# Opening of an attention + two-MLP kernel: pair 0's q and k loaded half from each queue, and its single-head score tiles read unstacked operands

## The chip, the cores and the metric

The kernel runs on one core of one Trainium2 chip. The metric is the device time of one execution in microseconds (us); the time before is the median of three executions. One further execution was recorded by the hardware profiler, and all rows below come from it. Engines are named as in the profile: PE (TensorE matmuls), PEld (its weight loads), DVE (VectorE), ACT (ScalarE), POOL (GpSimd), SP (SyncE); SPq and ACTq are rows in which SP and ACT issue DMAs.

## The reference

```python
q, k, v: (4, 8, 576, 64)          # batch, heads, sequence, head dim
scores = 64 ** -0.5 * q @ k.T
thresh = max(scores) - tau
scores = where(scores >= thresh, scores, -1e9)
attn = exp(scores - max(scores)); attn /= sum(attn) + 1e-9
x = (attn @ v), heads side by side -> (2304, 512)
h = x @ w_in;  x = (s * relu(h) ** 2 + b) @ w_out          # 512 -> 2048 -> 512
h = x @ w_in2; out = (max(h, 0) + alpha * min(h, 0)) @ w_out2
```

All inputs and outputs are float32.

## The kernel before

**Precision.** Every matrix product is made of three matmuls in a fast float32 form: each operand is split in a high and a low part (`q_hi`, `q_lo`, ...), and hi·hi, lo·hi and hi·lo are accumulated in PSUM.

**Attention.** The 32 heads go in 16 pairs. One pair has nine score tiles of 128 queries by 576 keys: tiles 0 to 7 alternate between the two heads (`t.i`, with `t.head = t.i % 2`), and tile 8 (`t.of_both`, `FULL = 8`) holds the last 64 queries of both. A pair is laid out over twelve steps, `LAYOUT = ["Q", 0, 1, "K", 2, 3, "L", 4, 5, 6, 7, 8]`. At step Q PE transposes the raw q of the next pair, and ACT and DVE write `q_hi` and `q_lo`; step K does it for k; at step L the last tile of the pair before is turned. A tile goes PE (`fill`), DVE maximum (`row_max`, L788), ACT exponential (L616), DVE threshold and sum (`mask`, L796), which frees the PSUM slot. Three wide PSUM slots are used in rotation, so tile 4 of pair 0 waits for the mask of tile 2, tile 5 for that of tile 3, tile 7 for that of tile 4, tile 8 for that of tile 5, and the first tile of pair 1 for that of tile 7. POOL normalises, PE turns the normalised rows (L1038) and multiplies by v (L1072).

**Stacked and unstacked scores.** One head has only 64 rows of contraction. `fill_scores` (L967, L969) does a half tile with two matmuls of 128 rows: `q_both` and `k_twice` hold hi and lo parts above each other, and `q_pad` holds `q_hi` of one head beside zeros. These stacked copies are made by DMA inside SBUF: `stack(n, par)` on SP, eleven DMAs counted by `stacked` (`STACK = 11`) and two for `q_diag_lo` counted by `diagonal`. `fill_scores_unstacked` does a half tile with three matmuls of 64 rows straight from `q_hi`, `q_lo`, `k_hi`, `k_lo` (L938, L939, L940). In pair 0 tiles 0 to 3 are unstacked (`OPENING = 4`); tile 8 always reads `q_pad` and `q_diag_lo`.

**What sets the order.** Each engine's program is written in order, and semaphores tie them. SP's program in the opening is: load q of pair 0, tau, q and k of pair 1, `stack(0, 0)`, `stack(1, 1)`, then the loads of pairs 2 and 3. ACT starts with the load of k of pair 0 and issues v of pairs 0 and 1 and q of pair 2 between its exponentials. PE runs 14 idle transposes (`run_idle`, L1077), then waits for all seven memsets of DVE (`padded`) and for q of pair 0.

**MLPs.** After the attention, two MLP layers run over five token tiles and keep PE busy to the end; the change does not touch them.

Of the kernel before, what the change touches and what calls it, by code (L numbers as in the profile page):

```python
# [26 lines left out]
F32 = mybir.dt.float32  # L27
# [5 lines left out]
P = 128  # L33
BANK = 512
DMA = 16


def attention_mlp_mlp(nc, q, k, v, tau, w_in1, w_out1, s, b, w_in2, w_out2, alpha, out):
    B, H, S, D = q.shape
# [6 lines left out]
    LAST = S - (QT - 1) * P  # L46
# [3 lines left out]
    FULL = 2 * (QT - 1)  # L50
# [12 lines left out]
    q_pairs = q.rearrange("b (n h) s d -> (b n) h s d", h=2)  # L63
    k_pairs = k.rearrange("b (n h) s d -> (b n) h s d", h=2)
    v_pairs = v.rearrange("b (n h) s d -> (b n) h s d", h=2)

    with ExitStack() as whole, ExitStack() as attention_memory:
# [14 lines left out]
        raw_q = sb("raw_q", [P, 2, QT, P], where=fetched)  # L82
        raw_k = sb("raw_k", [P, 2, QT, P], where=fetched)
# [13 lines left out]
        q_hi = sb("q_hi", [P, 2, S], F32R, att)  # L97
        q_lo = sb("q_lo", [P, 2, S], F32R, att)
# [5 lines left out]
        q_pad = sb("q_pad", [P, 2, 2 * S], F32R, att)  # L104

        q_diag_lo = sb("q_diag_lo", [P, 2, P], F32R, att)
# [40 lines left out]
        q_in = [sem(f"q_in{i}") for i in range(2)]  # L147
        k_in = [sem(f"k_in{i}") for i in range(2)]
        v_in = [sem(f"v_in{i}") for i in range(2)]
        diagonal = [sem(f"diagonal{i}") for i in range(2)]  # L150
# [43 lines left out]
        def wait_alone(eng, sm, value):  # L194

            if not (isinstance(value, int) and value <= 0):
                eng.wait_ge(sm, value)
                eng.sem_inc(tick, 1)
# [60 lines left out]
        def static(x):  # L259
            return isinstance(x, int)  # L260
# [112 lines left out]
        block = whole.enter_context(nc.Block())  # L373


        def load(eng, raw, par, pairs, n, order, landed):

            for h in range(2):
                eng.dma_start(raw[:, par, 0:QT - 1, D * h:D * h + D],
                             pairs[bass.ds(n, 1), h, 0:S - LAST, :].rearrange(order, p=P)  # L380
                             ).then_inc(landed, DMA)

        def load_tails(eng, raw, par, pairs, n, landed):
            eng.dma_start(raw[0:LAST, par, QT - 1, :].rearrange("p (h d) -> p h d", h=2),
                         pairs[bass.ds(n, 1), :, S - LAST:S, :].rearrange("o h p d -> p (o h) d")
                         ).then_inc(landed, DMA)

        def load_raw_q(eng, n, par):
            load(eng, raw_q, par, q_pairs, n, "o (t p) d -> p (o t) d", q_in[par])
            load_tails(eng, raw_q, par, q_pairs, n, q_in[par])  # L390

        def load_raw_k(eng, n, par):
            load(eng, raw_k, par, k_pairs, n, "o (p t) d -> p (o t) d", k_in[par])
            load_tails(eng, raw_k, par, k_pairs, n, k_in[par])
# [13 lines left out]
        @block.sync  # L408
        def _(sp):
            def load_qk(n, par):  # L410
                if not (static(n) and n < 2):
                    wait_alone(sp, filled, k_filled(n - 2))
                load_raw_q(sp, n, par)
                load_raw_k(sp, n, par)

            def q_filled(n):

                return 1 if static(n) and n == 0 else Use(n - 1, Q_POS).uses + 1

            def k_filled(n):  # L420

                return 2 if static(n) and n == 0 else Use(n - 1, K_POS).uses + 1

            def stack(n, par):

                def put(dst, src, landed=stacked):
                    sp.dma_start(dst.bitcast(F32), src.bitcast(F32)).then_inc(landed[par], DMA)

                a, b, most, rest = slice(0, D), slice(D, P), slice(0, S - LAST), slice(S - LAST, S)
                wait_alone(sp, qk_hi_ok, 2 * n + 1)  # L430
                put(q_both[a, par, 0, :], q_hi[a, par, most])
                put(q_both[b, par, 1, :], q_hi[b, par, most])
                if static(n) and n == 0:
                    sp.wait_ge(padded, PADDED)
                    sp.wait_ge(diag_padded, 1)
                put(q_pad[a, par, 0:S], q_hi[a, par, :])
                put(q_pad[b, par, S:S + LAST], q_hi[b, par, rest])
                put(q_pad[b, par, S + LAST:2 * S], q_hi[b, par, most])
                wait_alone(sp, freed, q_filled(n))
                put(q_both[b, par, 0, :], q_lo[a, par, most])  # L440
                put(q_both[a, par, 1, :], q_lo[b, par, most])
                wait_alone(sp, qk_hi_ok, 2 * n + 2)
                for rows in (a, b):
                    put(k_twice[rows, par, 0, :], k_hi[a, par, LAST:S + LAST])
                    put(k_twice[rows, par, 1, :], k_hi[b, par, 0:S])
                put(q_diag_lo[a, par, 0:D], q_lo[a, par, rest], diagonal)
                put(q_diag_lo[b, par, D:P], q_lo[b, par, rest], diagonal)

            def load_v(n, par):
                wait_alone(sp, pv_done, 2 * (n - 1))  # L450
                load_raw_v(sp, n, par)

            def load_w_in1(n):
                sp.dma_start(win_raw[:, :, bass.ts(n, P)], in_chunk(w_in1, n)).then_inc(win_in, DMA)

            def in_chunk(w, n):
                return w[:, bass.ts(n, P)].rearrange("(c p) f -> p c f", p=P)

            load_raw_q(sp, 0, 0)
            sp.dma_start(tau_c[:], tau.partition_broadcast(P)).then_inc(tau_in, DMA)  # L460
            load_raw_q(sp, 1, 1)
            load_raw_k(sp, 1, 1)
            stack(0, 0)
            stack(1, 1)
            sp.wait_ge(filled, k_filled(0))
            load_raw_k(sp, 2, 0)
            load_qk(3, 1)
            with sp.Fori(1, PAIRS // 2 - 1) as it:
                for par in range(2):
                    n = it * 2 + par  # L470
                    stack(n, par)
                    load_qk(n + 2, par)
                    load_w_in1(n)
                    load_v(n, par)
            for n in range(PAIRS - 2, PAIRS):
                stack(n, n % 2)
                load_w_in1(n)
                load_v(n, n % 2)
                load_w_in1(n - (PAIRS - 2))
            sp.dma_start(s_c[:], s.partition_broadcast(P)).then_inc(const_in, DMA)  # L480
            sp.dma_start(b_c[:], b.partition_broadcast(P)).then_inc(const_in, DMA)
            sp.dma_start(alpha_rows[:], alpha.rearrange("(j p) -> j p", p=P)).then_inc(const_in, DMA)
            sp.wait_ge(filled, k_filled(PAIRS - 1))
            for number, m in enumerate(STAGED):
                kind, j = WEIGHTS[m]
                slot = number % 4
                if number >= 4:
                    sp.wait_ge(w_ok, STAGED[number - 4] + 1)
                dst = stage[:, slot, :]
                if kind == "in2":  # L490
                    sp.dma_start(dst.rearrange("p (c f) -> p c f", c=DC), in_chunk(w_in2, j)).then_inc(stage_in[slot], DMA)
                else:
                    src = w_out1 if kind == "out1" else w_out2
                    sp.dma_start(dst, src[j * P:(j + 1) * P, :]).then_inc(stage_in[slot], DMA)

            def store(i):
                for sub in range(subs(i)):
                    wait_alone(sp, y_ok[sub], i + 2)
                    sp.dma_start(out[bass.ds(i * TOK + sub * P, P), :], y_sb[:, sub, :]).then_inc(y_out[sub], DMA)

            with sp.Fori(0, FULL_TILES) as i:
                store(i)
            store(FULL_TILES)
            for sub in range(SUB):
                sp.wait_ge(y_out[sub], DMA * (1 + FULL_TILES + (sub < REST_SUB)))
# [67 lines left out]
        def _(act):  # L573
# [107 lines left out]
                    load_raw_v(act, 1, 1, [V1_AT.index(l)])  # L681

            V0_AT, Q2_AT, V1_AT = [0, 1, 2], 3, [5, 6, 7]
            load_raw_k(act, 0, 0)
            act.wait_ge(ident_ok, 2)
            nc.scalar.activation(one_exp[:], ident[:, 0:1], ACT.Exp)
            steps(act, emit)
# [247 lines left out]
        def _(pe):  # L935
# [34 lines left out]
                                              start=False, stop=True)  # L970
                mm.then_inc(filled, 1)

            OPENING, QUIET = 4, 4

            def fill_scores_unstacked(t):
                lhs = [x[t.part, t.parity, t.q0:t.q0 + P] for x in (q_hi, q_lo)]
# [101 lines left out]

            pe.wait_ge(ident_ok, 2)
            run_idle(14)  # L1080
            pe.wait_ge(padded, PADDED)

            def emit(n0, l):
                for back in (l % POS, l % POS + POS):
                    t = Use(n0, l - back)
                    if t.inside:
                        for group, c in PV.get(back, ()):
                            times_v(t.pair, t.parity, group, c)
                fill(Use(n0, l + 2), n0, l + 2)
                if static(n0) and n0 == 0 and l < QUIET:  # L1090
                    run_idle(3)
                for t in turns_at(n0, l):
                    turn(t)
# [111 lines left out]
```

## Time and profile before

| | us |
|---|---|
| median of 3 runs | 1107.29 (1106.79 to 1107.41) |
| profiled execution, its own time | 1107.03 |
| span of the profiled execution | 1105.1 |
| PE busy | 1090.8 (99% of the span) |
| DVE busy | 525.6 |
| mean granted TensorE clock | 0.998 of full speed |

The span runs from the first instruction to the last. The profile gives the busy time of each engine, a chain of waits followed back from the last instruction, and, for a stretch, the instructions of each engine in order of time, with the idle time before each and what ended it. Starts are in us from the span's start.

### The profile page before, as it was taken

The numbers are of one execution on the slowest core, as the hardware profiler recorded it, in microseconds if no ns is written. First come the engines' busy times: TensorE is split into PE (matmuls) and PEld (weight loads), VectorE is DVE, ScalarE is ACT, GpSimd is POOL, SyncE is SP. The second block draws the span as 40 slices with busy tenths as digits, with TensorE's granted clock in tenths as the row PEclk, the third lists the DMA queues.
The fourth block names the chain that finished last, engine by engine and source line by source line (L and its number), as shares of the span: only waits on it lengthen the run. The fifth ranks groups of instructions, "written<-read, shape, count | busy, mean of one in ns | idle before, by whom it ended". The sixth has DMA issues, their size and how long they took to land.

```text
span 1105.1 us, 18966 instructions
## 1 busy us (share of the span) xinstructions
PE 1090.8 (99%) x5826; PEld 892.2 (81%) x5826; DVE 525.6 (48%) x1016; ACT 507.9 (46%) x946; POOL 258.0 (23%) x438
## 2 busy tenths in 40 slices
PE   8999999999999999999999999999999999999998
PEld 7777877777688888888888889888888888888897
DVE  7888889888643332242242246522322332332232
ACT  4777878777654332232232235544433333333343
POOL 3566656566564300000000004322000000000000
PEclk9999999999999999999999999999999999999999
DMA  8666566664121100000000003311100100010010
GB/s 188 153 157 154 141 150 149 153 146 123 31 58 48 48 1 1 1 0 0 0 0 0 0 10 96 86 48 29 39 0 0 38 0 0 0 38 0 0 39 20
DMA packets 86554, 59.28 MB, mean 54 GB/s; under 512 B 49376, under 2 KB 69872, under 8 KB 86512
## 3 DMA queue, kind: packets, MB, share of 16 engines
q1 hardware_dynamic: 83248, 57.58, 20.5%
q10 hardware_dynamic: 3264, 1.18, 0.5%
q8 instruction: 22, 0.36, 0.1%
q14 instruction: 20, 0.16, 0.1%
HBM read 30.94 MB, written 4.72 MB: 32 GB/s over the span
## 4 chain that ended last, share of the span: by engine, by line
PE 93%; DVE 2%; ACT 2%; issue 1%; DMA 0%; POOL 0%; SPq 0%; ACTq 0%; POOLq 0%; DVEq 0%
PE psum L938 23%; PE psum L940 23%; PE psum L939 23%; PE psum L1072 6%; PE psum L1038 5%; PE psum L967 3%; PE psum L969 3%; PE psum L951 2%; PE psum L1067 2%; DVE act_r L874 2%; PE psum L1046 1%; ACT win_hi L593 1%; PE psum L1035 1%; ACT act_r L706 0%; DMA k_twice<-k_hi 0%
## 5 line engine op out<-in xcount | busy, mean ns | idle before, releaser
L940 PE MATMUL psum<-x_hi,win_lo 128*128 128x512 f32 (+1 forms) x640 | 238.7, 373 | 0.0
L939 PE MATMUL psum<-x_lo,win_hi 128*128 128x512 f32 (+1 forms) x640 | 238.2, 372 | 0.0
L938 PE MATMUL psum<-x_hi,win_hi 128*128 128x512 f32 (+1 forms) x640 | 238.1, 372 | 0.0
L939 PEld LDWEIGHTS psum<-x_lo,win_hi 128*128 128x128 f32 x640 | 120.2, 188 | 24.0
L938 PEld LDWEIGHTS psum<-x_hi,win_hi 128*128 128x128 f32 x640 | 120.3, 188 | 23.0
L940 PEld LDWEIGHTS psum<-x_hi,win_lo 128*128 128x128 f32 x640 | 120.2, 188 | 22.9
L885 DVE SCALAR_TENSOR_TENSOR act_r<-act_n,nalpha,act_r 128x512 f32<-128x512 f32 (+1 forms) x80 | 56.2, 702 | 160.1 <-ACT act_r L717 159.8
L874 DVE SCALAR_TENSOR_TENSOR act_r<-act_r,s_c 128x512 f32<-128x512 f32 (+1 forms) x80 | 72.4, 905 | 116.4 <-ACT act_r L706 116.4
L616 ACT ACTIVATE ex<-psum,negm 128x576 f32<-128x576 f32 x144 | 107.5, 747 | 37.9 <-DVE negm L788 36.7
L709 ACT ACTIVATE g_hi<-act_r,b_c 128x512 fp32r<-128x512 f32 (+1 forms) x80 | 54.6, 682 | 152.5 <-PE psum L940 122.4
L550 POOL TENSOR_SCALAR ex<-ex,none_in,rinv 128x576 f32<-128x576 f32 x142 | 117.5, 828 | 19.9 <-DVE rinv L807 13.0
L796 DVE SCALAR_TENSOR_TENSOR ex<-psum,thr,ex 128x576 f32<-128x576 f32 x144 | 117.1, 813 | 8.8 <-ACT ex L616 3.7
L788 DVE TENSOR_REDUCE negm<-psum 128x1 f32<-128x576 f32 x144 | 107.8, 748 | 25.7 <-PE psum L969 24.1
L877 DVE SCALAR_TENSOR_TENSOR g_lo<-act_r,b_c,g_hi 128x512 fp32r<-128x512 f32 (+1 forms) x80 | 56.4, 704 | 133.6 <-ACT g_hi L709 133.6
L938 PE MATMUL psum<-g_hi,wout_hi 128*128 128x512 f32 (+1 forms) x320 | 118.1, 369 | 1.0 <-DVE g_lo L877 1.0
L940 PE MATMUL psum<-g_hi,wout_lo 128*128 128x512 f32 (+1 forms) x320 | 118.1, 369 | 0.0
L939 PE MATMUL psum<-g_lo,wout_hi 128*128 128x512 f32 (+1 forms) x320 | 117.7, 368 | 0.0
L940 PE MATMUL psum<-wout_hi,g_lo 128*128 128x512 f32 x288 | 112.6, 391 | 0.0
L938 PE MATMUL psum<-wout_hi,g_hi 128*128 128x512 f32 x288 | 112.4, 390 | 0.0
L939 PE MATMUL psum<-wout_lo,g_hi 128*128 128x512 f32 x288 | 112.2, 390 | 0.0
L888 DVE TENSOR_TENSOR g_lo<-act_r,g_hi 128x512 fp32r<-128x512 f32 (+1 forms) x80 | 51.1, 639 | 105.8 <-ACT g_hi L720 105.8
L716 ACT ACTIVATE act_n<-psum 128x512 f32<-128x512 f32 (+1 forms) x80 | 44.3, 554 | 120.7 <-PE psum L940 120.7
(93 smaller groups left out, 1614.7 us busy)
## 6 DMA issues: line engine op xcount, KB each, us to landing
k_twice<-k_hi SPq DMA_DIRECT2D x64, 144.0 KB, 2.5
stage<-in_moe_w_out_dram SPq DMA_DIRECT2D x32, 256.0 KB, 2.6
out_dram<-stage SPq DMA_DIRECT2D x18, 256.0 KB, 2.2
q_both<-q_hi SPq DMA_DIRECT2D x32, 128.0 KB, 2.3
q_both<-q_lo SPq DMA_DIRECT2D x32, 128.0 KB, 2.3
win_raw<-in_moe_w_in_dram SPq DMA_DIRECT2D x16, 256.0 KB, 2.9
stage<-in_moe_w_in_dram SPq DMA_DIRECT2D x16, 256.0 KB, 2.6
raw_q<-in_q_dram SPq DMA_DIRECT2D x30, 128.0 KB, 2.4
```

The costliest lines, as they stand in the source:

```text
L550: nc.gpsimd.tensor_scalar(t.ex, t.ex, none_in[r, c], rinv[r, c], ALU.add, ALU.mult).then_inc(normed, 1)
L616: nc.scalar.activation(t.ex.rearrange("p (a c) -> p a c", a=2), t.wide[r, :, 0:HALF], ACT.Exp, bias=negm[r, t.col]).then_inc(exped, 1)
L788: nc.vector.tensor_reduce(negm[r, t.col], t.wide[r, :, 0:HALF], AX.XY, ALU.max, negate=True).then_inc(maxed, 1)
L796: nc.vector.scalar_tensor_tensor(out=e, in0=t.wide[r, :, 0:HALF], scalar=thr[r, t.col], in1=e, op0=ALU.is_ge, op1=ALU.mult, accum_out=rsum ...
L874: nc.vector.scalar_tensor_tensor(out=r, in0=r, scalar=s_c[:], in1=r, op0=ALU.mult, op1=ALU.mult).then_inc(t_ok, 1)
L877: nc.vector.scalar_tensor_tensor(out=g_lo[:, j % 2, 0:n], in0=r, scalar=b_c[:], in1=g_hi[:, j % 2, 0:n].bitcast(F32), op0=ALU.add, op1=ALU ...
L885: nc.vector.scalar_tensor_tensor(out=r, in0=act_n[:, j % 2, 0:n], scalar=nalpha[:, j:j + 1], in1=r, op0=ALU.mult, op1=ALU.add).then_inc(t_ ...
L938: nc.tensor.matmul(dst, lhs[0], rhs[0], start=first, stop=False)
L939: nc.tensor.matmul(dst, lhs[0], rhs[1], start=False, stop=False)
L940: return nc.tensor.matmul(dst, lhs[1], rhs[0], start=False, stop=final)
L1038: mm = nc.tensor.transpose(t.buf[:, c, :], ex[:, t.keys0 + c * P:t.keys0 + (c + 1) * P], ident[:])
L1072: nc.tensor.matmul(o_bank[part, o_cols], raw_v[:, par, h, c, :], pt[:, h, c, cols], start=(c == 0), stop=False)
```

## The change

1. **Loads of pair 0.** SP loads head 0 of q, q's tails and head 0 of k; ACT loads head 1 of q, head 1 of k and k's tails. Before, SP had all of q and ACT all of k.
2. **Scores of pair 0.** `OPENING = FULL`, so tiles 0 to 7 are all unstacked.
3. **Stack of pair 0.** Nothing reads `q_both` and `k_twice` of pair 0 any more. `short_stack` issues four DMAs of 64 columns for tile 8, two into `q_pad` and two into `q_diag_lo`, and adds the missing nine increments to `stacked` itself.
4. **PE's first wait.** PE waits for two memsets before the first transposes, and for all seven only before tile 0.

```diff
+        def load_first(eng, head, of_q=True):
+            if of_q:
+                load(eng, raw_q, 0, q_pairs, 0, "o (t p) d -> p (o t) d", q_in[0], [head])
+            else:
+                load(eng, raw_k, 0, k_pairs, 0, "o (p t) d -> p (o t) d", k_in[0], [head])
...
+            def short_stack():
+                rest = slice(S - LAST, S)
+                sp.wait_ge(padded, PADDED)
+                sp.wait_ge(diag_padded, 1)
+                for part, col in ((slice(0, D), S - LAST), (slice(D, P), S)):
+                    sp.dma_start(q_pad[part, 0, col:col + LAST].bitcast(F32),
+                                 q_hi[part, 0, rest].bitcast(F32)).then_inc(stacked[0], DMA)
+                sp.sem_inc(stacked[0], (STACK - 2) * DMA)
+                sp.wait_ge(freed, q_filled(0))
+                for h in range(2):
+                    part = slice(D * h, D * h + D)
+                    sp.dma_start(q_diag_lo[part, 0, part].bitcast(F32),
+                                 q_lo[part, 0, rest].bitcast(F32)).then_inc(diagonal[0], DMA)
...
                 wait_alone(sp, qk_hi_ok, 2 * n + 1)
+                if static(n) and n == 0:
+                    short_stack()
+                    return
                 put(q_both[a, par, 0, :], q_hi[a, par, most])
                 put(q_both[b, par, 1, :], q_hi[b, par, most])
-                if static(n) and n == 0:
-                    sp.wait_ge(padded, PADDED)
-                    sp.wait_ge(diag_padded, 1)
...
-            load_raw_q(sp, 0, 0)
+            load_first(sp, 0)
+            load_tails(sp, raw_q, 0, q_pairs, 0, q_in[0])
+            load_first(sp, 0, False)
...
-            load_raw_k(act, 0, 0)
+            load_first(act, 1)
+            load_first(act, 1, False)
+            load_tails(act, raw_k, 0, k_pairs, 0, k_in[0])
...
-            OPENING, QUIET = 4, 4
+            OPENING, QUIET = FULL, 4
...
             run_idle(14)
-            pe.wait_ge(padded, PADDED)
+            pe.wait_ge(padded, 2)
 
             def emit(n0, l):
+                if static(n0) and n0 == 0 and l == 0:
+                    pe.wait_ge(padded, PADDED)
```

On SP, between the loads of pair 1 and the loads of pair 2, the program before has both full stacks (a put is L427; the semaphores waited for stand in brackets):

```order
L427 DMA q_both<-q_hi 64x512 [waits qk_hi_ok]
L427 DMA q_both<-q_hi 64x512
L427 DMA q_pad<-q_hi 64x576 [waits diag_padded,padded]
L427 DMA q_pad<-q_hi 64x64
L427 DMA q_pad<-q_hi 64x512
L427 DMA q_both<-q_lo 64x512 [waits freed]
L427 DMA q_both<-q_lo 64x512
L427 DMA k_twice<-k_hi 64x576 [waits qk_hi_ok]
L427 DMA k_twice<-k_hi 64x576 x3
L427 DMA q_diag_lo<-q_lo 64x64 x2
L427 DMA q_both<-q_hi 64x512 [waits qk_hi_ok]
```

and the changed program has, in the same place:

```order
L437 DMA q_pad<-q_hi 64x64 [waits qk_hi_ok,diag_padded,padded]
L437 DMA q_pad<-q_hi 64x64
L443 DMA q_diag_lo<-q_lo 64x64 [waits freed]
L443 DMA q_diag_lo<-q_lo 64x64
L449 DMA q_both<-q_hi 64x512 [waits qk_hi_ok]
```

The last row of each is the first put of pair 1: it moves from behind thirteen DMAs to behind four.

On PE, the program before has tiles 4 and 5 of pair 0 as four matmuls each, the first of them behind `stacked0`:

```order
L967 MATMUL psum<-k_twice,q_both 128x288 [waits stacked0,freed]
L969 MATMUL psum<-k_lo,q_pad 128x288
L967 MATMUL psum<-k_twice,q_both 128x288
L969 MATMUL psum<-k_lo,q_pad 128x288
L967 MATMUL psum<-k_twice,q_both 128x288 [waits freed]
```

and the changed program has tile 4 and the first matmul of tile 5 as:

```order
L964 MATMUL psum<-k_hi,q_hi 128x288 [waits freed]
L965 MATMUL psum<-k_lo,q_hi 128x288
L966 MATMUL psum<-k_hi,q_lo 128x288
L964 MATMUL psum<-k_hi,q_hi 128x288
L965 MATMUL psum<-k_lo,q_hi 128x288
L966 MATMUL psum<-k_hi,q_lo 128x288
L964 MATMUL psum<-k_hi,q_hi 128x288 [waits freed]
```

Each of tiles 4 to 7 has two matmuls more, and the wait on `stacked0` has moved to tile 8.

## Rows read from the trace of the kernel before

**Rows 1.** The page: span, busy tenths of PE, granted clock, in 40 slices.

```profile
span 1105.1 us, 18966 instructions
...
PE   8999999999999999999999999999999999999998
...
PEclk9999999999999999999999999999999999999999
```

**Rows 2.** Stretches: start:end, length; busy PE, PEld, DVE, ACT, POOL; clock; DMA.

```profile
2.00:4.00 2.00, 2.00 (x12) 2.00 (x11) 1.70 (x2) 0.48 (x1) 0.00 (x0) 1.00 0.95 215
...
14.10:17.50 3.40, 2.59 (x17) 1.85 (x16) 3.15 (x8) 1.14 (x3) 1.32 (x3) 1.00 1.04 252
17.50:20.90 3.40, 3.04 (x12) 2.92 (x12) 2.73 (x8) 1.25 (x2) 1.55 (x4) 0.51 1.12 224
20.90:24.30 3.40, 2.52 (x18) 2.02 (x17) 3.40 (x9) 2.33 (x4) 2.34 (x5) 0.99 1.11 240
24.30:27.70 3.40, 2.37 (x20) 1.96 (x19) 2.88 (x10) 3.19 (x6) 2.51 (x7) 1.00 0.69 153
...
28.00:30.00 2.00, 2.00 (x18) 1.81 (x17) 1.79 (x5) 1.50 (x4) 0.98 (x4) 1.00 0.69 153
```

**Rows 3.** The chain of waits in the opening: start, us, what.

```profile
22.76 4.51 DMA k_twice<-k_hi
...
27.41 0.37 PE psum L967
```

**Rows 4.** Timeline of SP's DMA issues: start, us, engine, what, count.

```profile
11.58 2.46 SPq L427 DMA_DIRECT2D k_twice<-k_hi  x4
...
15.62 1.17 SPq L427 DMA_DIRECT2D q_both<-q_hi  x2
```

**Rows 5.** Timeline of the head: PE's weight loads and ACT's last load of k.

```profile
1.54 2.85 PEld L1077 LDWEIGHTS psum<-ident 128*128 128x128 f32 x14 [1.54 <-POOL ident L512]
...
2.72 0.77 ACTq L384 DMA_DIRECT2D raw_k<-in_k_dram  x1
...
4.84 0.93 PEld L951 LDWEIGHTS psum<-ident,raw_q 128*128 128x128 f32 x5 [0.46 <-issue]
...
6.40 1.14 PEld L951 LDWEIGHTS psum<-ident,raw_k 128*128 128x128 f32 x6
```

**Rows 6.** Timeline of ACT writing the high parts of pair 1.

```profile
9.11 0.65 ACT L627 ACTIVATE q_hi<-psum 128x576 fp32r<-128x576 f32 x1 [0.50 <-PE psum L951]
...
13.57 0.69 ACT L627 ACTIVATE k_hi<-psum 128x640 fp32r<-128x640 f32 x1
```

**Rows 7.** Timeline of DVE's maxima (L788) and masks (L796) from tile 3 on.

```profile
18.05 0.82 DVE L796 SCALAR_TENSOR_TENSOR ex<-psum,thr,ex 128x576 f32<-128x576 f32 x1 [0.24 <-ACT ex L616]
...
19.23 0.76 DVE L788 TENSOR_REDUCE negm<-psum 128x1 f32<-128x576 f32 x1 [0.35 <-PE psum L969]
...
20.30 0.76 DVE L788 TENSOR_REDUCE negm<-psum 128x1 f32<-128x576 f32 x1
20.97 0.81 DVE L796 SCALAR_TENSOR_TENSOR ex<-psum,thr,ex 128x576 f32<-128x576 f32 x1
...
25.34 0.81 DVE L796 SCALAR_TENSOR_TENSOR ex<-psum,thr,ex 128x576 f32<-128x576 f32 x1
...
28.21 0.76 DVE L788 TENSOR_REDUCE negm<-psum 128x1 f32<-128x576 f32 x1 [1.00 <-PE psum L969]
```

**Rows 8.** Timeline of PE: two matmuls of tile 3, then tiles 4 and 5.

```profile
15.53 0.29 PE L940 MATMUL psum<-k_hi,q_lo 64*128 64x288 f32 x1
15.66 0.29 PE L938 MATMUL psum<-k_hi,q_hi 64*128 64x288 f32 x1
...
17.86 0.61 PE L967 MATMUL psum<-k_twice,q_both 128*128 128x288 f32 x1 [1.17 <-DVE ex L796]
...
18.74 0.45 PE L969 MATMUL psum<-k_lo,q_pad 128*128 128x288 f32 x1
...
18.98 0.55 PE L967 MATMUL psum<-k_twice,q_both 128*128 128x288 f32 x1
```

More of the change, by code:

```diff
@@ L373, in attention_mlp_mlp, with load @@
         block = whole.enter_context(nc.Block())
-        def load(eng, raw, par, pairs, n, order, landed):
-            for h in range(2):
+        def load(eng, raw, par, pairs, n, order, landed, heads=range(2)):
+            for h in heads:
                 eng.dma_start(raw[:, par, 0:QT - 1, D * h:D * h + D],
```

## The prediction

> **What bounds the kernel now.** I read the page first: PE is eight or nine tenths busy in every slice of the 40 and its clock is full [rows 1]. So the kernel is bound by PE, and a change to the opening is worth the time by which PE's unbroken stretch starts earlier. The view by stretches shows where that begins: from 28 us on PE works 2.00 of 2.00, while from 24.3 to 27.7 it works 2.37 of 3.40 [rows 2]. The chain of waits names what holds it last: the last `k_twice` put of pair 1 takes 4.51 us from 22.76 to its landing, and the first tile of pair 1 starts behind it at 27.41 [rows 3]. The put is late because SP issues thirteen puts for pair 0 first; pair 1's first goes out at 15.62 [rows 4]. DVE is the other engine to watch: it sits idle 1.00 us before that tile's maximum at 28.21, but from 20.9 to 24.3 it works 3.40 of 3.40 [rows 2, 7].
>
> One more thing stands in the stretches, TensorE's clock: 0.51 of full from 17.5 to 20.9, so the level of 1.2 GHz, and 2.4 GHz on both sides [rows 2]. Tiles 4 and 5 and most of tile 6 fall in it. There the matmuls of a tile follow each other by 0.24 us (18.74 to 18.98), at the full level by 0.13 us (15.53 to 15.66) [rows 8].
>
> **The change part by part.** The sum is made against the profiled execution: 1107.03 us, which is the span of 1105.1 and 1.9 around it, and 0.26 below the median of 1107.29.
>
> *Head (loads of pair 0, PE's first wait).* The weight loads of PE's idle transposes end at 1.54 + 2.85 = 4.39, and q's first weights load at 4.84, 0.46 us of idleness later [rows 5]. Two waits can end there, the memsets of DVE and the landing of q's tails. Both get shorter: PE needs two memsets only, and q's tails become SP's second issue instead of its third. So q starts up to 0.45 us earlier. For k nothing improves: its tails remain ACT's third issue, at 2.72, and k's weights load at 6.40 with no idleness before them, which says only that k had landed by then [rows 5]. Bounds: nothing, if k's landing takes over at once (or a loss as small, if the interleaved loads delay k), and 0.45 if all passes through. I take 0.25, near the middle, as neither row speaks for an end.
>
> The DMA engines are already 0.95 busy from 2 to 4 us [rows 2]. The Trainium skill has a rule that speaks against this part ("DMA: Bandwidth & Descriptors", "Issuing engines are not separate DMA queues"): transfers started from several engines share the same DMA engines and save only the time of issuing. The busy share agrees. By the rule alone the split is worth nothing more than q's tails issued earlier; with no gain in the head at all the forecast would be 1106.9 instead of 1106.6.
>
> *Stack of pair 0.* Thirteen puts become four. The first put of pair 1 needs `q_hi` of pair 1, done at 9.11 + 0.65 = 9.8 [rows 6]; four puts at 0.6 each (2.46 for four [rows 4]) are out before that. So it goes out 5.8 us earlier. Pair 1's `k_twice` puts need `k_hi`, done at 13.57 + 0.69 = 14.3 [rows 6], so they are out by 14.3 + 2.46 = 16.8 and landed, even at the 4.51 of [rows 3], by 21.3. PE asks for them past 26. The wait goes with 5 us to spare, and SP's later loads move up too. What is late next: PE's own transposes before the tile, over at 27.41 - 1.03 = 26.4 (3.40 - 2.37 = 1.03 idle [rows 2]), and DVE's mask of tile 7, which frees the slot at 25.34 + 0.81 = 26.15 [rows 7]. Gain on both engines: 1.0 us.
>
> *Tiles 4 to 7 unstacked.* Eight matmuls more. Tile 4 starts at 17.86, released by DVE's mask of tile 2 and not by the stack [rows 8], so it starts no earlier but for the head. At half clock its six matmuls occupy PE until 17.86 + 0.40 + 5 x 0.24 = 19.46 (0.40 for the first, as now: 18.98 - 17.86 less 3 x 0.24), where tile 5 now starts at 18.98. Tile 5's last matmul starts at 19.46 + 5 x 0.24 = 20.66 and ends 0.45 later, at 21.1, so DVE's maximum of tile 5 moves from 20.30 to 21.14, by 0.84 [rows 7]. From there DVE works without a stop to the last mask of pair 0, so all of it shifts by 0.84, the mask of tile 7 too. Tiles 6 and 7 run at full clock again; their extra matmuls, 2 x 0.13 each, lie beside DVE's 0.76 + 0.81 per tile. With tiles 4 and 5 at full clock the price would be nothing for the same reason. That is the lower bound; the upper one is below under B. I take 0.84, since nothing in the change removes the idle time ahead of the half-clock stretch.
>
> *Sum:* -0.25 - 1.0 + 0.84 = -0.4 us, so 1107.03 - 0.4 = 1106.6.
>
> **Rivals.**
> A. *No half clock in pair 0.* For it: PE has more matmuls to do from 18 on, and the gap before 17.86 may shrink. Against it: that gap, 1.17 us, hangs on DVE's masks [rows 8]. Price: the maximum of tile 4 starts when DVE has finished mask 3, at 18.05 + 0.82 = 18.87 instead of 19.23; the maximum of tile 5 follows it at once, and the mask of tile 4 comes at 20.3 instead of 20.97 [rows 7]. DVE is unbroken from there, so 0.67 earlier. Sum: -0.25 - 1.0 - 0.67 = -1.9, so 1105.1.
>
> B. *More half clock, and slower than before.* The clock fell at 17.5, behind a stretch in which PE did tiles 2 and 3 as 64-row matmuls and then stood idle; it did not fall behind 20.9 to 24.3 or 24.3 to 27.7, where PE worked no more (2.52 and 2.37 against 2.59) but with 128-row matmuls [rows 2, 8]. The change puts 64-row matmuls in tiles 4 to 7. So the level of 1.2 GHz may last for another stretch, or come back. From 20.9 to 24.3 DVE, with 3.40 of 3.40, hides most of it: the time is about that of before. It decides when it covers the transposes and tiles from 24.3 on, where PE is what others wait for: 3.4 us at half speed lose 1.7. Sum: -0.4 + 1.7 = +1.3, so 1108.3; twice that, 1110. The Trainium skill ("TensorE: Matmul & The Clock Gate", "What's actually happening") says that the low level is the default and that activity lifts it; it says nothing there on 64 rows. By that sentence alone the added matmuls would speak for A; the three stretches just compared speak for B.
>
> C. *The wait doesn't turn into time.* The tile starts earlier, but the turning of pair 0 is then held by POOL, which normalises tiles 7 and 8 behind the threshold of pair 1's first tile. For it: DVE feeds POOL and is nearly full. Against it: that threshold moves up with the tile. The same time results if the new load order delays k, or if `short_stack` sits in SP's queue longer than reckoned. Sum: +0.0 to -0.25, so 1106.8 to 1107.3.
>
> **How the numbers follow.** The forecast 0.48 (its own range 1106.1 to 1107.2), A 0.17, B 0.20, C 0.15. What a measurement of this kernel can tell from no change is about 0.2%, 2.2 us, so "within" is 1105.1 to 1109.5. Only A with the full head gain of 0.45 passes the lower bound; with something for gains that I don't see, faster by over 0.2% has 0.12. Only B with two stretches passes the upper: 0.05. Within has 0.83. The range goes from A less a tenth, 1105.0, to B and a little more, 1108.6.
>
> **What would show it.** In the profile after: q's first weights at 4.4 to 4.6, k's at 6.1 to 6.4; SP's first put of pair 1 near 9.8 and its last `k_twice` out by 17; no wait of PE on `k_twice`; tile 4 as six matmuls from about 17.6 on, 0.24 us apart, and DVE's maximum of tile 5 near 20.9; one half-clock stretch of about 3.4 us, and the first tile of pair 1 near 27.0 instead of 27.41. That tile near 25.5, and no half clock, means A; near 28 or later, with a second half-clock stretch, B. The forecast is wrong outright if the first maximum of pair 1 moves by over 2 us either way, or if PE's rows after 28 us show waits that they don't have now.

## The result and the profile after

The changed kernel has a median of 1109.21 us (1107.51 to 1109.9, 17 runs) against 1106.9 (1106.55 to 1108.7, 17 runs) for the kernel before: a ratio of 1.0018, 95% interval 1.0011 to 1.0024. By that ratio it is slower by 2.0 us (1.2 to 2.7); the medians lie 2.3 apart. The forecast was 1106.6 in a range that ended at 1108.6, so both its sign and its range were wrong. The profiled execution took 1108.34 us, 1.3 more than that of before, so most executions lost more than the one whose rows follow.

The stretches of the changed kernel, in the columns of [rows 2], show where it went:

```profile
16.00:18.00 2.00, 1.05 (x6) 0.81 (x6) 1.68 (x6) 0.74 (x1) 1.55 (x3) 1.00 1.12 210
18.00:20.00 2.00, 1.97 (x11) 1.98 (x12) 1.10 (x4) 0.74 (x1) 0.67 (x3) 0.50 1.12 217
20.00:22.00 2.00, 1.07 (x5) 0.72 (x4) 2.00 (x5) 0.74 (x1) 1.70 (x3) 0.50 1.16 231
22.00:24.00 2.00, 2.00 (x11) 1.72 (x9) 1.51 (x6) 0.74 (x1) 0.27 (x1) 0.50 1.32 211
24.00:26.00 2.00, 2.00 (x11) 1.98 (x10) 1.15 (x6) 1.23 (x2) 1.30 (x3) 0.50 0.51 107
26.00:28.00 2.00, 2.00 (x11) 2.00 (x10) 1.90 (x5) 1.23 (x2) 1.22 (x3) 0.50 0.35 79
28.00:30.00 2.00, 2.00 (x17) 1.79 (x16) 1.30 (x4) 1.53 (x4) 0.89 (x2) 0.94 0.01 4
```

The last number but two is the clock. It is 0.50 from 18 to 28 us, ten microseconds where the profile of before had 3.4. From 22 to 28 PE is busy without a gap, at half speed. DVE works 1.51 and 1.15 of 2.00 from 22 to 26, where it was full in the kernel before:

```profile
22.00:24.00 2.00, 1.80 (x13) 1.56 (x14) 2.00 (x6) 1.29 (x3) 1.29 (x3) 1.00 1.10 226
24.00:26.00 2.00, 2.00 (x18) 1.79 (x17) 2.00 (x5) 1.79 (x3) 1.41 (x4) 1.00 0.76 163
```

PE's timeline has the transposes and the first tile of pair 0, then tile 7, the end of tile 8 and the first tile of pair 1:

```profile
1.54 3.10 PE L1103 MATMUL psum<-ident 128*128 128x128 f32 x14 [1.54 <-POOL ident L536]
4.48 0.71 PE L977 MATMUL psum<-ident,raw_q 128*128 128x128 f32 x5
...
5.94 0.84 PE L977 MATMUL psum<-ident,raw_k 128*128 128x128 f32 x6 [0.42 <-DMA raw_k<-in_k_dram]
...
8.62 0.36 PE L964 MATMUL psum<-k_hi,q_hi 64*128 64x288 f32 x1 [0.31 <-DVE k_lo L840]
...
21.41 0.60 PE L964 MATMUL psum<-k_hi,q_hi 64*128 64x288 f32 x1 [0.93 <-DVE ex L822]
...
25.26 0.44 PE L966 MATMUL psum<-k_hi,q_diag_lo 128*128 128x288 f32 x1
25.50 1.05 PE L1064 MATMUL psum<-ident,ex 128*128 128x128 f32 x4
26.35 1.27 PE L977 MATMUL psum<-ident,raw_q 128*128 128x128 f32 x5
27.41 1.45 PE L1064 MATMUL psum<-ident,ex 128*128 128x128 f32 x8
28.62 0.38 PE L993 MATMUL psum<-k_twice,q_both 128*128 128x288 f32 x1
```

The first tile of pair 1 no longer waits for any DMA, yet it starts at 28.62 instead of 27.41 [rows 3]. DVE's maxima of tiles 5, 7 and 8 and of pair 1's first tile now wait for PE, where only the last did so before [rows 7]:

```profile
19.87 0.76 DVE L814 TENSOR_REDUCE negm<-psum 128x1 f32<-128x576 f32 x1 [0.86 <-PE psum L966]
...
23.25 0.76 DVE L814 TENSOR_REDUCE negm<-psum 128x1 f32<-128x576 f32 x1 [0.49 <-PE psum L966]
...
25.74 0.76 DVE L814 TENSOR_REDUCE negm<-psum 128x1 f32<-128x576 f32 x1 [0.85 <-PE psum L966]
...
29.45 0.76 DVE L814 TENSOR_REDUCE negm<-psum 128x1 f32<-128x576 f32 x1 [0.70 <-PE psum L995]
```

SP does what was forecast: pair 1's first put goes out at 9.92 instead of 15.62 [rows 4], its `k_twice` puts are out by 17.6.

```profile
9.92 1.16 SPq L449 DMA_DIRECT2D q_both<-q_hi  x2
...
14.61 2.94 SPq L449 DMA_DIRECT2D k_twice<-k_hi  x4
```

### The profile page after: what moved, and what is told of

Its sections match the earlier page's. It is cut to its first block, busy times and chain, and to the rows that moved or that the text cites. A ratio compares the mean times of both kernels' runs of the same rounds, so it can differ in the third digit from the quotient of the medians.

```text
span 1106.5 us, 18973 instructions
## 1 busy us (share of the span) xinstructions
PE 1092.6 (99%) x5834; PEld 894.3 (81%) x5834; DVE 526.1 (48%) x1016; ACT 507.7 (46%) x946; POOL 258.0 (23%) x438
## 4 chain that ended last, share of the span: by engine, by line
PE 93%; DVE 3%; ACT 2%; issue 1%; POOL 0%; DMA 0%; ACTq 0%; POOLq 0%; DVEq 0%
PE psum L964 23%; PE psum L966 23%; PE psum L965 23%; PE psum L1098 6%; PE psum L1064 5%; PE psum L993 3%; PE psum L995 3%; PE psum L977 2%; PE psum L1093 2%; DVE act_r L900 2%; PE psum L1072 1%; ACT win_hi L617 1%; PE psum L1061 1%; ACT act_r L732 0%; DMA raw_k<-in_k_dram 0%
```

## The experiments

For every run the mean granted clock over the whole span is known. A microsecond at half clock takes half a microsecond off it, so over 1107 us a mean of 0.995 is about 11 us at half clock (10 to 12, by the rounding), 0.998 about 4, and 1.0 about 1 or less; in the traces up to 1.4 us of it lie at the very end of the kernel (e4). The changed kernel had 0.995 or 0.996 in all 17 runs. The 33 runs of the kernel before that went with e1 to e4 had 0.996 or 0.997 in 13 and 0.998 or 1.0 in 20. The 13 took no longer than the others: the medians by clock lie between 1106.8 and 1107.0. So the kernel before, too, has more than 3.4 us of half clock in some runs, and there it costs nothing.

**The unstacked tiles alone (e1).** The kernel before with:

```diff
-            OPENING, QUIET = 4, 4
+            OPENING, QUIET = FULL, 4
```

> The kernel before with OPENING = FULL alone: pair 0's tiles 4 to 7 as six 64-row matmuls, all else (loads, eleven-DMA stack) as before. Theory 64-ROW: these tiles keep TensorE's clock at half level for about 10 us, as in the profile of the changed kernel; the wait on k_twice stays but is covered, so about 1109 to 1110 us (+2 to +3). Theory LOADS (the new load order disturbs the opening): same clock as before, one half-clock stretch of 3.4 us, about 1107.0 to 1107.8.

Measured: 1108.61 against 1106.95, ratio 1.0016 (1.0007 to 1.0025), mean clock 0.995 to 0.997. Its stretches show the same half clock as those of the changed kernel:

```profile
20.00:22.00 2.00, 1.07 (x6) 0.72 (x4) 1.83 (x4) 0.74 (x1) 1.69 (x3) 0.50 0.93 286
22.00:24.00 2.00, 2.00 (x9) 1.72 (x9) 1.51 (x4) 0.74 (x1) 0.46 (x2) 0.50 0.97 226
24.00:26.00 2.00, 2.00 (x10) 1.98 (x9) 1.19 (x5) 1.23 (x2) 1.08 (x3) 0.50 0.65 143
26.00:28.00 2.00, 2.00 (x11) 2.00 (x11) 1.93 (x4) 1.11 (x2) 1.23 (x3) 0.50 0.51 119
```

This one constant brings most of the loss, somewhat less than the 2 to 3 us expected.

**The loads alone (e2).** The kernel before with the diff's `load_first`, the new order of loads and PE's shorter first wait.

> The kernel before with the new load order and PE's shorter first wait alone. Theory 64-ROW: the first tile of pair 0 starts 0.3 to 1.0 us earlier, but the first tile of pair 1 still waits for k_twice, whose puts are bound by SP's queue; 1106.4 to 1107.0 (0 to -0.5), one half-clock stretch. Theory LOADS: slower than before by over 1 us, or the long half-clock stretch appears here too.

Measured: 1107.12, ratio 1.0005 (0.9995 to 1.0014). Seven runs lie at 1106.7 to 1107.3 with a clock of 0.997 to 1.0, four at 1108.0 to 1108.4 with 0.995. So neither text is right: the loads cost nothing clear of noise, but the half clock did get longer in some runs, and the four with the lowest clock are 1 us slower. In the profiled one, at 1107.04, it lasted 6.8 us, from 19.1 to 25.9, though tiles 4 to 8 have only 128-row matmuls here:

```profile
20.00:22.00 2.00, 1.00 (x5) 0.73 (x4) 1.93 (x5) 1.15 (x3) 1.51 (x5) 0.50 1.13 273
22.00:24.00 2.00, 2.00 (x11) 1.98 (x11) 2.00 (x5) 1.17 (x3) 1.12 (x3) 0.50 1.08 223
```

PE had stood idle for 2.06 us before tile 4 and for 1.00 before tile 7. So 64 rows are not the only thing that can go with a longer half clock. The profile also shows why starting pair 0 earlier gains nothing while its stack is whole: tile 4 is ready sooner and then waits 2.06 us for its own `k_twice`.

```profile
17.99 0.37 PE L978 MATMUL psum<-k_twice,q_both 128*128 128x288 f32 x1 [2.06 <-DMA k_twice<-k_hi]
```

**Rows or count (e3, e4).** Two kernels that change only tiles 4 to 7 of pair 0. e3 keeps four matmuls per tile and gives them 64 rows; it leaves out the product hi·lo of these tiles:

```diff
+                    if static(t.pair) and t.pair == 0 and not t.of_both:
+                        nc.tensor.matmul(dst, q_hi[t.part, t.parity, cols], k_hi[t.part, t.parity, k0:k0 + HALF],
+                                         start=True, stop=False)
+                        mm = nc.tensor.matmul(dst, q_hi[t.part, t.parity, cols], k_lo[t.part, t.parity, k0:k0 + HALF],
+                                              start=False, stop=True)
+                    elif t.of_both:
-                    if t.of_both:
```

> The kernel before, with pair 0's tiles 4 to 7 as two 64-row matmuls per half (hi.hi and lo.hi, read unstacked; the product hi.lo is left out) in place of two 128-row ones: as many matmuls of as many columns as before, at the same places and behind the same waits, only with 64 rows. Theory 64-ROW: the half-clock stretch grows from 3.4 us to 7 or 10 us, 1108 to 1109. Rival COUNT (it is the number of matmuls, or the time PE works, and not their rows): one stretch of 3.4 us and the time of before, 1106.9.

e4 has six matmuls of 128 rows:

```diff
+                        if static(t.pair) and t.pair == 0:
+                            nc.tensor.matmul(dst, q_both[:, t.parity, t.head, cols], k_twice[:, t.parity, t.head, keys],
+                                             start=True, stop=True)
                         nc.tensor.matmul(dst, q_both[:, t.parity, t.head, cols], k_twice[:, t.parity, t.head, keys],
                                          start=True, stop=False)
```

> The kernel before, with the first matmul of each half of pair 0's tiles 4 to 7 issued twice: six 128-row matmuls per tile, the number of the changed kernel. Theory 64-ROW: one half-clock stretch of 3.4 us; the two extra matmuls of tiles 4 and 5 at 0.24 us shift DVE by up to 0.84, which the 1.0 us wait on k_twice covers, so 1106.9 to 1107.3. Rival COUNT: long half clock and 1109.

Measured: e3 1107.54 us, ratio 1.0006 (0.9997 to 1.0015), clock 0.997 in seven runs and 0.995 in four; e4 1106.96, ratio 1.0000 (0.9991 to 1.0009), clock 0.998 or 1.0 in all eleven. The stretches of e3:

```profile
20.00:22.00 2.00, 0.43 (x5) 0.16 (x1) 1.90 (x6) 1.47 (x2) 1.36 (x4) 0.50 1.10 251
22.00:24.00 2.00, 2.00 (x9) 1.72 (x9) 1.99 (x6) 0.74 (x1) 1.25 (x3) 0.50 1.08 224
24.00:26.00 2.00, 2.00 (x10) 1.98 (x10) 1.15 (x5) 1.23 (x2) 1.31 (x3) 0.50 0.76 161
```

and of e4:

```profile
20.00:22.00 2.00, 2.00 (x11) 1.83 (x9) 1.56 (x5) 0.93 (x2) 1.06 (x3) 0.63 1.10 275
22.00:24.00 2.00, 1.50 (x12) 1.30 (x11) 2.00 (x6) 1.30 (x2) 1.56 (x4) 1.00 1.05 221
24.00:26.00 2.00, 2.00 (x16) 1.79 (x16) 2.00 (x6) 1.75 (x3) 0.80 (x3) 1.00 0.73 160
```

From 22 to 26 the first is at 1.2 GHz and the second at 2.4. Six matmuls per tile of 128 rows leave the clock no lower than before; four of 64 rows hold it down. COUNT falls. By times alone e3 would not settle it, as its interval reaches below 1; the clocks do. With six matmuls each, those of e1 and e4 (0.995 to 0.997 against 0.998 or 1.0) don't overlap. With four each, e3 has 0.995 or 0.997, and the kernel before 0.998 or 1.0 in 20 of 33 runs. Against e1, four instead of six matmuls also spare PE work while the clock is low, which may be why it is 1107.5 and not 1108.6 us; I had expected 1108 to 1109.

But e3 did not keep the matmuls at the same places, as its expectation says. Tiles 5 and 6 belong to the two heads, and their 64-row matmuls ran side by side on PE: the eight took 1.34 us (18.93 to 20.27), where the eight of 128 rows took 2.19. PE then stood idle for 1.57 us before tile 7, where the kernel before has 0.68:

```profile
18.93 0.62 PE L963 MATMUL psum<-k_hi,q_hi 64*128 64x288 f32 x2
...
21.84 0.60 PE L963 MATMUL psum<-k_hi,q_hi 64*128 64x288 f32 x1 [1.57 <-DVE ex L796]
```

So e3 and e4 differ in PE's idle time as well as in rows (0.43 and 2.00 us of work from 20 to 22), and e2 shows that a long half clock can go with idle time alone. What tells the two apart is the trace of the next kernel.

**The short stack without the loads (e8).** The changed kernel with the loads and the first wait of before.

> The changed kernel with the loads and PE's first wait of before: tiles 4 to 7 unstacked and the short stack alone. Against e1 (1108.6) it shows the worth of the short stack. Theory 64-ROW: DVE and PE are both behind where k_twice lands, so the short stack brings next to nothing: 1108.2 to 1108.8; and the changed kernel's 1109.2 against it is what the loads cost. Theory of the sum in the forecast: 1.0 us faster than e1, 1107.6.

Measured: 1109.08, ratio 1.0019 (1.0010 to 1.0028), a little above what either text expected, against 1108.61 of e1 and 1109.21 of the changed kernel. Taking thirteen DMAs down to four brings nothing measurable while the clock is low, and putting the loads back mends nothing. Whether the short stack costs some 0.4 us stays open: the intervals overlap. Its stretches, at the times of [rows 2], are the cleanest comparison for the clock:

```profile
17.50:20.90 3.40, 3.12 (x15) 2.84 (x16) 2.04 (x7) 1.23 (x2) 1.31 (x3) 0.50 1.12 229
20.90:24.30 3.40, 2.47 (x13) 2.12 (x11) 2.90 (x6) 1.73 (x3) 2.37 (x5) 0.50 1.03 199
```

Half clock begins at 17.4 here and at 17.6 in the kernel before, and from 17.5 to 20.9 PE is as busy in both (3.12 and 3.04 us). With 128 rows the clock was back at 21.0. With 64 rows it came back only at 27.7, though PE's next idle time began after 21.9. This is one trace against one, but with the 11 runs each of e1 and e4 it speaks for the rows and not for idle time.

**Holding the clock up (e5, e6, e7).** Idle transposes of 128 rows, whose result nobody reads, in PE's gaps: ten before tile 4 (`{4: 10}`) in e5 and e7, and three more before each of tiles 5, 6 and 7 in e6, whose edit is shown. e5 and e6 start from the changed kernel, e7 from the kernel before.

```diff
                 if static(n0) and n0 == 0 and l < QUIET:
                     run_idle(3)
+                if static(n0) and n0 == 0 and l in {4: 10, 5: 3, 6: 3, 7: 3}:
+                    run_idle({4: 10, 5: 3, 6: 3, 7: 3}[l])
```

> The changed kernel with ten idle 128-row transposes (about 1.1 us at full clock) in the gap of 1.17 us in which PE waits for the mask of tile 2, ahead of tile 4. Theory 64-ROW plus gap (the clock falls behind a stretch of 64-row matmuls and idleness, and stays down through tiles 4 to 7): the fall is avoided in most executions, mean clock 0.998 to 1.0 instead of 0.995, and about 1105.1 to 1106 us. Rival (the time of the changed kernel is lost to something else than the clock): no more than 0.3 us from 1109.

> As the last, and three more idle transposes after each of tiles 4, 5 and 6. Theory 64-ROW: these cover the waits before tiles 5 to 7 too; the clock stays at full in nearly all executions, 1105 to 1105.5 us. If ten transposes in the one gap are enough, it equals the last within 0.3. If the extra transposes stand in the way of the tiles, 0.5 to 1 slower than the last.

> The kernel before with the same ten idle transposes ahead of tile 4. The clock of tiles 4 to 6 is then full, DVE is 0.67 earlier, but the first tile of pair 1 waits for k_twice at 27.3 as before: 1106.6 to 1107.0, no faster than before by over 0.3. If it is faster by 1 us or more, the wait on k_twice is not what holds the kernel before.

Measured: e5 1108.35, ratio 1.0012 (1.0003 to 1.0021), clock mostly 0.997. The fall only moved, from 18.0 to 20.4 us, behind a stretch (18 to 20) in which PE worked 1.03 of 2.00. That expectation was too hopeful. e6: 1106.24, ratio 1.0005 (0.9994 to 1.0016); nine of twelve runs at 1105.9 to 1106.3 with a clock of 0.999 or 1.0, and three at 1109.2, 1111.4 and 1111.6 with 0.997 and twice 0.995. I had expected 1105 to 1105.5. Where the clock stays up, the changed kernel is 3 us faster than without the filling; of the three runs in which it fell, one took as long as the changed kernel and two took 2 us longer. No trace of such a run was kept; that the fillers themselves ran at half speed there is likely, not shown. e7: 1106.64, ratio 0.9999 (0.9990 to 1.0008): the kernel before gains nothing from a full clock. Its first tile of pair 1 then waits 1.7 us for the put:

```profile
PE psum L967 <- DMA k_twice<-k_hi: 1.7, 1, 1.7
```

So the change does remove a real wait. What that is worth with the loads can be read only roughly from e6 against e7, as e6 has nine idle transposes more: 0.4 us by medians, 0.9 between the runs with a clock of 1.0 (about 1106.2 and 1107.1). Both intervals hold 1, so neither is clear of noise.

**Mostly 128 rows (e9, e10).** The changed kernel with `q_pad` of pair 0 whole (five DMAs), and in tiles 4 to 7 two of three matmuls per half from it:

```diff
...
+                    for n, k in enumerate((k_hi, k_lo)):
+                        nc.tensor.matmul(dst, q_pad[:, 0, pad0:pad0 + P], k[:, 0, k0:k0 + HALF],
+                                         start=n == 0, stop=False)
+                    mm = nc.tensor.matmul(dst, lhs[1], rhs[0], start=False, stop=True)
...
```

> The changed kernel with one more DMA in the short stack (q_pad of pair 0 whole, five DMAs) and tiles 4 to 7 as hi.hi and lo.hi from q_pad, 128 rows, and only hi.lo with 64 rows: same number of matmuls as the changed kernel, four of six with 128 rows. Theory 64-ROW: the half-clock time falls from 10 us to 3.4 or 7 us, mean clock 0.997 to 0.998, 1107 to 1108 us. Rival (the short stack and the loads are what costs): 1109 as the changed kernel.

> The last with the idle transposes of e6 (ten before tile 4, three after each of tiles 4 to 6). Theory 64-ROW: mean clock 1.0 in nearly every run, 1106.0 to 1106.3, without e6's executions at 1109 to 1111.5.

Measured: e9 1112.59 (5 runs), ratio 1.0051 (1.0037 to 1.0065), far outside its expectation; e10, with e6's idle transposes, 1107.73, ratio 1.0006 (0.9997 to 1.0015), clock 0.999 or 1.0 in all runs but 1.5 us slower than expected. The timeline of e9 shows what I hadn't counted. One tile at full clock, and the start of one at half:

```profile
17.02 0.40 PE L1013 MATMUL psum<-k_hi,q_pad 128*128 128x288 f32 x1 [1.17 <-DVE ex L823]
17.26 0.29 PE L1013 MATMUL psum<-k_lo,q_pad 128*128 128x288 f32 x1
17.48 0.40 PE L1015 MATMUL psum<-k_hi,q_lo 64*128 64x288 f32 x1
17.81 0.40 PE L1013 MATMUL psum<-k_hi,q_pad 128*128 128x288 f32 x1
...
22.16 0.61 PE L1013 MATMUL psum<-k_hi,q_pad 128*128 128x288 f32 x1
22.57 0.44 PE L1013 MATMUL psum<-k_lo,q_pad 128*128 128x288 f32 x1
22.94 0.61 PE L1015 MATMUL psum<-k_hi,q_lo 64*128 64x288 f32 x1
23.48 0.61 PE L1013 MATMUL psum<-k_hi,q_pad 128*128 128x288 f32 x1
```

Each change between 128 and 64 rows holds PE up: a half tile takes 0.79 us (17.02 to 17.81) instead of 0.40 to 0.49, and 1.32 (22.16 to 23.48) instead of 0.72 to 0.89 at half clock (the larger number is for a tile's first half). The clock, at half from 18.4 to 32.0 us here, didn't come back any sooner, though four of six matmuls had 128 rows and PE counts as busy throughout from 20 to 32. So e9 doesn't test what it was made for, and the row theory rests on e1, e4 and e8. e10 has the same half tiles at full clock: 1.5 us more than e6's median.

**A second thing in the way (e12, e13).** In e6 DVE waits 1.57 us for the exponential of tile 3:

```profile
18.51 0.82 DVE L822 SCALAR_TENSOR_TENSOR ex<-psum,thr,ex 128x576 f32<-128x576 f32 x1 [1.57 <-ACT ex L640]
```

because ACT first issues q of pair 2, which took long, beside SP's puts on the other queue:

```profile
14.72 2.18 ACTq L379 DMA_DIRECT2D raw_q<-in_q_dram  x2
```

```profile
14.38 3.12 SPq L449 DMA_DIRECT2D k_twice<-k_hi  x4
```

In the kernel before the same four puts took 2.46 us for pair 0 [rows 4]. That the queues slow each other is not shown by this. In the profile of the changed kernel the same two issues start together, at 14.61, and ACT's takes 1.01 us:

```profile
14.61 1.01 ACTq L379 DMA_DIRECT2D raw_q<-in_q_dram  x2
```

What made the difference stays open. e12 is e6, and e13 is e10, with:

```diff
-            V0_AT, Q2_AT, V1_AT = [0, 1, 2], 3, [5, 6, 7]
+            V0_AT, Q2_AT, V1_AT = [0, 1, 2], 4, [5, 6, 7]
```

> e6 (changed kernel, all gaps filled) with ACT's load of q of pair 2 issued one step later, behind the exponential of tile 3 instead of ahead of it. In e6 the issue took 0.75 + 2.18 us, beside SP's k_twice puts at 14.4 to 17.5, and DVE waited 1.57 us for that exponential. Theory ISSUE (this is the second thing that ate the gain): the wait goes, the chain is 1.0 to 1.4 us earlier, 1104.9 to 1105.3 us where the clock stays up. Rival (something else is late by then): 1106.2 as e6.

> e10 with the same later load of q of pair 2. Both theories together: 1104.9 to 1105.3 us, in nearly every execution; 2 us faster than the kernel before.

Measured: e12 1105.90 against 1107.10, ratio 0.9992 (0.9983 to 1.0001), clock 0.999 or 1.0 in all eleven runs, 1105.6 to 1106.6. DVE's wait has shrunk to 0.18 us:

```profile
17.24 0.82 DVE L822 SCALAR_TENSOR_TENSOR ex<-psum,thr,ex 128x576 f32<-128x576 f32 x1 [0.18 <-ACT ex L640]
```

It is 0.34 faster than e6's median, not the 1.0 to 1.4 I had expected. Of the 1.27 us by which the mask of tile 3 is earlier (17.24 against 18.51), the first maximum of pair 1 keeps 0.82 (26.60 against 27.42) and the profiled executions 0.48; I did not find where the rest went. e12 also shows none of e6's three runs with a low clock. It is the best kernel of the study, 3.3 us below the changed one by medians, and probably 1 us below the kernel before, though its interval just touches no change. e13, expected at 1104.9 to 1105.3: 1107.65, ratio 1.0005 (0.9996 to 1.0014), no faster than e10, whose half tiles it has.

## Why the prediction was wrong

**What bounds the kernel** was right. The loss arose before 30 us: the first tile of pair 1 is 1.2 us later, the profiled execution 1.3 us longer, and from 28 to 445 us PE is as busy as before (412.8 us before, 412.7 after).

**Head: q right, k not.** q's transposes start at 4.48, as forecast. k's start at 5.94 and wait 0.42 us for k's landing. The forecast was that nothing improves for k, at 6.1 to 6.4; but in e1, which has the old loads and also waits for that landing, they start at 6.27, so k lands 0.33 us sooner. The first tile starts at 8.62 instead of 9.61, and not all of that is the loads. The traces differ in the pace of PE's first transposes (five of q took 1.30 us before, 0.71 after), which the granted clock, 1.00 throughout up to 10 us, doesn't show. Where the five took 0.71 to 0.79 us, the first tile is at 8.62 (changed) and 8.79 (e9) with the new loads and at 8.95 (e1, e4) with the old ones; where they took 1.21 to 1.30, at 8.72 to 9.19 with the new and 9.55 to 9.72 with the old. So the loads gave 0.2 to 0.3 us in the one case, as forecast (0.25), and 0.4 or more in the other.

**Stack of pair 0: right, but worth nothing here.** The put leaves at 9.92 (forecast 9.8), and no wait on `k_twice` is left. The 1.0 us that this freed is seen, if at all, only where the clock is full (e6 against e7: 0.4 to 0.9, not clear of noise). Beside a low clock e1 and e8 don't differ by more than their intervals.

**Tiles 4 to 7 unstacked: the step that failed.** The words were "Tiles 6 and 7 run at full clock again". The term of +0.84 rested on a half-clock stretch that stays as it was, with only two tiles in it. In the profile after it lasts from 18 to 28 us. Then tile 7, tile 8, two turnings, the transposes of q and two more turnings, from 21.41 to 28.62, run at half speed on PE without a gap, and PE takes DVE's place as the bound. They take 7.21 us; the kernel before needed 4.55 for them (21.84 to 26.39). Of the 2.66 us, the end of the wait on `k_twice` gives 1.03 back and the earlier start of tile 7 0.43; the rest is the 1.2 us by which the tile is late.

The 0.84 itself did not come either. The maximum of tile 5 was to move from 20.30 to 21.14, and came at 19.87. Tile 4 fell outside the half-clock stretch this time (its maximum came at 17.98, 1.25 earlier than before), and tiles 5 and 6 were worked out as matmuls 0.24 us apart, while the second half of tile 5 and the first of tile 6 ran side by side. (With tile 5's own pace before, its last matmul at 19.82, four more at 0.24 would have been 0.96.) So by 20 us the changed kernel was ahead, and lost it after. e1 shows that this term alone is most of the loss, e4 and e8 that it goes with the 64 rows. How a mix of heights acts (e9), and how much idle time adds (e2), stays open.

**The rivals.** B had the mechanism, the place and the direction: it named PE's work from 24.3 us on as what decides. It was given 0.20. The profile has two stretches of 3.4 us more, for which its price was 1110, and took 1108.34; its price for one, 1108.3, is short of the median. So a stretch was priced too high. I had the three stretches in hand that spoke for it (2.59 us of PE work with 64 rows and the clock fell, 2.52 and 2.37 with 128 rows and it held) and still kept the stretch as a constant in the sum. A is what e6 shows where the clock holds, at 1106.2 instead of the 1105.1 worked out; ACT's long issue of q of pair 2 explains about the 0.3 us that e12 gained, and the rest stays open. C could not show in this kernel, as the tile did not start earlier. The sentence of the Trainium skill that activity lifts the low level ("TensorE: Matmul & The Clock Gate", "What's actually happening") did not help to choose. In the changed kernel PE had more matmuls but was busy for less time from 18 to 22 us, 3.04 instead of 3.32, which doesn't speak against it; in e8 PE was as busy as before, and the clock stayed low all the same.

## What to carry to other kernels

A term of a sum that depends on TensorE's clock is not a constant: when a change alters what PE does just before or in a half-clock stretch, above all when full-height matmuls become 64-row ones with idle gaps between, price the case that the stretch grows over everything that PE does next. A wait on a DMA that ends 1 us after all else is worth at most that 1 us, and the cheaper path that removes it must not slow the engine that becomes the bound. Idle work of full height in PE's gaps can hold the clock, but has to fill all gaps of the passage: one filled gap moved the fall by 2.4 us, four avoided it in 9 runs of 12, and 2 of the other 3 were slower than without fillers.

## What the runs showed of the hardware

- Matmuls of 64 rows hold the clock less well than those of 128. With six per tile the mean clock was 0.995 to 0.997 with 64 rows (e1) and 0.998 or 1.0 with 128 (e4), eleven runs each; and with PE equally busy (3.12 and 3.04 of 3.40 us) half clock lasted from 17.4 to 27.7 us with 64 rows (e8) and from 17.6 to 21.0 with 128 (the kernel before).
- 128 rows are no guarantee: behind idle times of 2.06 and 1.00 us half clock lasted 6.8 us with them (e2).
- 64-row matmuls of the two heads, on different halves of the partitions, run side by side: eight took 1.34 us at half clock (e3), where eight of 128 rows took 2.19.
- Switching between 128-row and 64-row matmuls holds PE up: a half tile of two and one took 0.79 us at full clock, where three alike take 0.40 to 0.49.
- The time to issue the same DMAs varies: ACT's two loads of q took 1.01 us in the changed kernel and 2.18 in e6, both beside four puts on SP's queue, which took 2.94 and 3.12 us and 2.46 in the kernel before. The cause was not found.
